# Dense stage of a three-stage kernel: first product two steps ahead of the second, row scaling in two parts, counts tile by tile

## The chip, the cores and the metric

The kernel runs on one core of one Trainium2 chip. The metric is the device time of one execution in microseconds (us). A core has a matrix engine (TensorE, PE in the rows), a vector engine (VectorE, DVE), a scalar engine (ScalarE, ACT), a general one (GpSimd, POOL) and queues for transfers; each runs its own list of instructions in order, and they wait for each other by semaphores. A bank is one of eight accumulator areas that TensorE writes.

## The reference

Three parts follow each other: a gated linear recurrence over 768 positions for 4 x 8 heads, a mixture of eight experts (top one), and a dense layer. The change touches only the last:

```python
def _moe2_ref(x, w_in, w_out) -> np.ndarray:      # x (3072, 320), w_in (320, 2048), w_out (2048, 320)
    h = x @ w_in
    g = np.maximum(0.01 * h, h)
    return (g @ w_out).astype(np.float32)
```

Its input is the experts' output, and its result is the output of the whole, 3072 rows of 320 float32 numbers.

## The kernel before

**Numbers in two halves.** Products are made with float16 operands. A float32 operand is split in a high half (its float16 rounding) and a low half (the rest), and three of the four partial products are summed in a bank: high by high, high by the weights' low half, low by high. Rows of x are first divided by a power of two of their size, so that halves keep their bits, and the result is multiplied by its inverse (`yinv`) at the end.

**Tiles and steps.** The 3072 rows are 24 tiles of 128 rows, in 6 groups (`NGR`) of 4 tiles (`GT`). The 2048 hidden columns are 16 steps (`2 * NF`) of 128. In a step f of a group:

- TensorE, `f_first`: first product, 8 matmuls over 512 columns (the group's rows), into `bank[f % 2]`; the rows say L1514.
- ACT, `group`: 0.01 times the bank into `ft` (L856).
- DVE, `group`: maximum of bank and `ft` into `fgl` (L1315).
- ACT: high half `fhi` from `fgl` (L860).
- DVE: low half `flo`, `fgl` minus `fhi` (L1320).
- TensorE, `f_second`: second product, for each of the 4 tiles 3 matmuls over 320 columns, summed over all steps in `bank[4]` to `bank[7]` (L1649).

`ft`, `fgl`, `fhi` and `flo` have two buffers each, by f % 2. In the traces' names `ft`, `fgl`, `yh`, `yl` and `ob` lie in "stage", `fhi` in "dec", `flo` and the scaled rows `ysc` in "qk".

**Order.** It is written by hand on each engine. TensorE issues first product f and then second product f - 1. At the border of two groups the last second product of the old group comes behind first product 0 of the new. After the last second product of a group ACT copies the four banks out with `rows_out` (L873, four instructions, one wait ahead of them), and the second product of step 0 waits for all four. POOL then scatters each tile's rows to the output by an indirect transfer (L627).

**Preparing the next group.** While group gr runs, the four tiles of group gr + 1 are made ready at the steps of `PREP_AT`: DVE's `y_scale` (L1295 to L1300: the rows' largest magnitude, five on one number per row, and two that scale the rows) stands between the maximum and the low half of step f; in the next step TensorE transposes the tile (`y_turn`, L1625, 3 matmuls) behind the second product, ACT takes the high half (`y_high`, L847) and DVE the low half (`y_low`, L1305). The last group has no such work.

**Counts.** `f_h`, `f_t`, `f_g`, `f_hi`, `f_lo` and `f_o` count first products, leaky parts, maxima, high halves, low halves and second products; `f_ob` counts output rows, by tiles.

Of the kernel before, what the change touches and what calls it, by code (L numbers as in the profile page):

```python
# [26 lines left out]
I32 = mybir.dt.int32  # L27
U32 = mybir.dt.uint32
ALU = mybir.AluOpType
ACT = mybir.ActivationFunctionType  # L30
AX = mybir.AxisListType
ds = bass.ds
# [14 lines left out]
NPAIR = NST + NE - 1  # L47
KR = DM - 2 * P
NF = FE // P
NU = NE + 2  # L50
GT = 4
NGR = NST // GT
# [3 lines left out]
POW_X = 2.0  # L56
# [8 lines left out]
def build(nc, qkT, k_in, v_in, o_in, ig, fg, wg_in, wA, wB, out):  # L65
    ctx = ExitStack()
    with ctx:
# [128 lines left out]
        m_h, m_hh, m_hl, m_o, m_y = sem("m_h"), sem("m_hh"), sem("m_hl"), sem("m_o"), sem("m_y")  # L196

        ys_chain, ys_done, f_tr, f_yh, f_yl = sem("ys_chain"), sem("ys_done"), sem("f_tr"), sem("f_yh"), sem("f_yl")
# [52 lines left out]
        Y = xreg[:, :].rearrange("p (t d) -> p t d", t=NST)  # L251
# [6 lines left out]
        sxt = sb("sxt", [P, 8], F32)  # L258
# [22 lines left out]
        def part(s, k):  # L281
# [1 line left out]
            if k < 3:  # L283
                return stA[s][:, k * FE:(k + 1) * FE]
            return stB[s][:, (k - 3) * NF // 2 * DM:(k - 2) * NF // 2 * DM]

        def pow2(dve, link, src, sc, inv, top):

            link(nc.vector.tensor_scalar(sc, src, 1e-30, 1e30, ALU.max, ALU.min))
            link(nc.vector.tensor_scalar(sc.bitcast(I32), sc.bitcast(I32), 0x7F800000, None, ALU.bitwise_and))  # L290
            nc.vector.tensor_scalar(inv, sc, 1.0 / top, None, ALU.mult)
            link(nc.vector.reciprocal(sc, sc))
            return nc.vector.tensor_scalar(sc, sc, top, None, ALU.mult)


        def row_of(eng, x):

# [337 lines left out]
        def _(act):  # L635
            a = nc.scalar
# [213 lines left out]
            def group(gr, i, prep):  # L850
                for f in range(2 * NF):
                    n = gr * 2 * NF + f
                    act.wait_ge(f_h, n + 1)
                    if not (isinstance(n, int) and n < 2):
                        act.wait_ge(f_g, n - 1)
                    a.activation(ft[f % 2], bank[f % 2][:, :], ACT.Copy, scale=0.01).then_inc(f_t, 1)  # L856
                    act.wait_ge(f_g, n + 1)
                    if not (isinstance(n, int) and n < 2):
                        act.wait_ge(f_o, n - 1)
                    a.copy(fhi[f % 2], fgl[f % 2]).then_inc(f_hi, 1)  # L860
                    if f == 0 and not (isinstance(gr, int) and gr == 0):
                        rows_out(gr - 1, 1 - i)
                    if prep and f - 1 in PREP_AT:
                        q = PREP_AT.index(f - 1)
                        y_high((gr + 1) * GT + q, 1 - i, q)

            def rows_out(gr, i):

                act.wait_ge(f_o, (gr + 1) * 2 * NF)
                if gr >= 2:  # L870
                    act.wait_ge(ob_free[i], 16 * GT // 2 * (gr - i))
                for q in range(GT):
                    a.activation(ob[i][:, q * DM:(q + 1) * DM], bank[4 + q][:, 0:DM], ACT.Copy,  # L873
                                 scale=yinv[:, ds(gr * GT + q, 1)]).then_inc(f_ob, 1)

# [8 lines left out]
        def _(dve):  # L884
# [397 lines left out]


            def y_scale(t, q):
                if not (isinstance(t, int) and t < 2):
                    dve.wait_ge(f_tr, t - 1)
                k = [0]

                def lk(ins):
                    k[0] += 1  # L1290
                    ins.then_inc(ys_chain, 1)
                    dve.wait_ge(ys_chain, t * YS_LINKS + k[0])

                yt = Y[:, ds(t, 1), :].rearrange("p a d -> p (a d)")
                lk(v.tensor_reduce(sxt[:, 0:1], yt, AX.X, ALU.max, apply_absolute_value=True))  # L1295
                lk(pow2(dve, lk, sxt[:, 0:1], sxt[:, 1:2], sxt[:, 2:3], POW_X))
                v.tensor_scalar(ysc[q % 2][:, 0:DM], yt, sxt[:, 1:2], None, ALU.mult)
                v.tensor_scalar(ysc[q % 2][:, DM:3 * P], Y[:, ds(t, 1), 2 * P:DM].rearrange("p a d -> p (a d)"),
                                sxt[:, 1:2], None, ALU.mult)
                v.tensor_tensor(yinv[:, ds(t, 1)], sxt[:, 2:3], winvp[:, NE:NE + 1], ALU.mult).then_inc(ys_done, 1)  # L1300
                assert k[0] == YS_LINKS, k[0]
# [7 lines left out]
            def group(gr, i, prep):  # L1309
                for f in range(2 * NF):  # L1310
                    w = gr * 2 * NF + f
                    dve.wait_ge(f_t, w + 1)
                    if not (isinstance(w, int) and w < 2):
                        dve.wait_ge(f_lo, w - 1)
                    v.tensor_tensor(fgl[f % 2], bank[f % 2][:, :], ft[f % 2], ALU.max).then_inc(f_g, 1)  # L1315
                    if prep and f in PREP_AT:
                        q = PREP_AT.index(f)
                        y_scale((gr + 1) * GT + q, q)
                    dve.wait_ge(f_hi, w + 1)
                    v.tensor_tensor(flo[f % 2], fgl[f % 2], fhi[f % 2], ALU.subtract).then_inc(f_lo, 1)  # L1320
                    if prep and f - 1 in PREP_AT:
                        q = PREP_AT.index(f - 1)
                        y_low((gr + 1) * GT + q, 1 - i, q)


# [23 lines left out]
        def _(pe):  # L1349
# [288 lines left out]
            def f_second(gr, f):  # L1638
                w = gr * 2 * NF + f
                pe.wait_ge(f_lo, w + 1)  # L1640
                if f == 0:
                    if isinstance(gr, int) and gr == 0:
                        pe.wait_ge(m_y, NPAIR + 1)
                    else:
                        pe.wait_ge(f_ob, gr * GT)
                for q in range(GT):
                    for z, (x, hl_) in enumerate(((fhi, 0), (fhi, 1), (flo, 0))):
                        c0 = (2 * (f % NF) + hl_) * DM
                        ins = t_.matmul(bank[4 + q][:, 0:DM], x[f % 2][:, q * P:(q + 1) * P],  # L1649
                                        slotB[2 + f // NF][:, c0:c0 + DM], start=(f == 0 and z == 0),  # L1650
                                        stop=(f == 2 * NF - 1 and z == 2))
                ins.then_inc(f_o, 1)

            def group(gr, i, prep):
                for f in range(2 * NF):
                    f_first(gr, f, i)
                    if f == 0 and not (isinstance(gr, int) and gr == 0):
                        f_second(gr - 1, 2 * NF - 1)
                    if f:
                        f_second(gr, f - 1)  # L1660
                    if prep and f - 1 in PREP_AT:
                        q = PREP_AT.index(f - 1)
                        y_turn((gr + 1) * GT + q, q)


# [12 lines left out]
                group(gr, 1, True)  # L1678
                group(gr + 1, 0, True)
            group(NGR - 1, 1, False)  # L1680
            f_second(NGR - 1, 2 * NF - 1)

# [12 lines left out]
NSL = 5  # L1697
XS_LINKS = 4
YS_LINKS = 5
PREP_AT = [2, 5, 8, 11]  # L1700
IN_PER_STEP = 16 * 8
HALF_ROW, BIG_ROW = -(P / 2 - 0.25), P * 1.5 * 2.0 ** 23

# [124 lines left out]
```

## Time and profile before

| | us |
|---|---|
| Median of three runs (lowest, highest) | 857.47 (855.05, 863.86) |
| The profiled execution, its own time | 860.35 |
| Its span in the trace | 858.6 |
| TensorE busy, page | 754.0 |
| First product of the dense stage starts | 497.15 |
| Last second product of the stage starts | 844.61 |

The page shows one execution. Busy time of matmuls is modelled: each is given a latency, so neighbours overlap in the rows, and the distance of two starts is what one costs. A row of the timeline has start and length in us, engine, line, operation, output and inputs, and in brackets how long the engine was idle before it and what ended that idleness. Rows of a list of waits have the total wait, how often, and the longest. The granted clock is given as a share of full speed.

### The profile page before, as it was taken

The page shows a single profiled execution, that of the slowest core. Times are in us where ns is not written, and L with a number is a line of the kernel's source. Part 1 is how long each engine was busy: PE and PEld are TensorE (multiplying, and loading weights), DVE is VectorE, ACT ScalarE, POOL GpSimd, SP SyncE. Part 2 cuts the span into 40 slices and gives each one's busy share as a digit, 9 for nine tenths or more (in the row PEclk, how much of TensorE's full clock was granted, in tenths as well). Part 3 has the DMA queues.
Part 4 walks back from the last instruction along what each step waited for, and adds up shares of the span by engine and source line. Part 5 has one row for each costly group of instructions (what it writes and reads, how often), then busy time and mean ns, then how long its engine had stood idle before and what let it go on. Part 6 is the DMA issues. An engine that isn't in the chain of part 4 may idle for free.

```text
span 858.6 us, 17692 instructions
## 1 busy us (share of the span) xinstructions
PE 754.0 (88%) x6435; PEld 553.7 (64%) x6436; DVE 535.2 (62%) x1406; ACT 391.2 (46%) x713; POOL 146.7 (17%) x202
## 2 busy tenths in 40 slices
PE   0789999998278899999999899999999999999993
PEld 0577887886167788888888755555555555555552
DVE  6468998896957556765567745455455454454341
ACT  2457474572526366554546233343433433434331
POOL 4334343443031111111100000010100100100101
PEclk9999999999589899999999999999999999999998
DMA  9569999991063983679420000000000000000000
GB/s 237 136 163 304 286 302 304 272 236 60 0 197 140 358 294 111 232 256 349 136 73 2 2 1 1 1 32 1 23 9 1 31 0 0 31 0 1 32 1 31
DMA packets 49401, 99.75 MB, mean 116 GB/s; under 512 B 7822, under 2 KB 38222, under 8 KB 46766
## 3 DMA queue, kind: packets, MB, share of 16 engines
q1 hardware_dynamic: 39906, 67.65, 26.4%
q10 hardware_dynamic: 6780, 22.10, 7.5%
q0 software_dynamic: 2640, 9.01, 3.1%
q8 instruction: 46, 0.75, 0.4%
q14 instruction: 29, 0.24, 0.1%
HBM read 74.85 MB, written 23.89 MB: 115 GB/s over the span
## 4 chain that ended last, share of the span: by engine, by line
PE 69%; DVE 12%; issue 7%; DMA 4%; ACT 4%; SPq 1%; POOL 1%; DVEq 0%; ACTq 0%
PE bank L1514 26%; PE bank L1649 13%; PE bank L1548 11%; PE bank L1381 4%; PE bank L1410 4%; ACT stage L856 2%; DVE qk L1320 2%; DMA vv<-v_in 2%; PE bank L1402 1%; PE bank L1394 1%; PE bank L1433 1%; DMA d_parts<-xreg 1%; DVE stage L1315 1%; DVE sxt L1295 1%; PE bank L1504 1%
## 5 line engine op out<-in xcount | busy, mean ns | idle before, releaser
L1514 PE MATMUL bank<-stage,slot 128*128 128x512 f16 x768 | 181.3, 379 | 0.0
L1649 PE MATMUL bank<-slot,dec 128*128 128x320 f16 x768 | 159.3, 299 | 15.7 <-DVE qk L1320 13.0
L1514 PE MATMUL bank<-qbd,slot 128*128 128x128 f16 x1984 | 122.3, 225 | 11.9 <-issue 11.7
L1315 DVE TENSOR_TENSOR stage<-bank,stage 128x512 f32<-128x512 f32 x96 | 66.4, 692 | 105.2 <-ACT stage L856 98.3
L1514 PEld LDWEIGHTS bank<-qbd,slot 128*128 128x128 f16 x1984 | 118.2, 101 | 15.4 <-issue 15.0
L1514 PEld LDWEIGHTS bank<-stage,slot 128*128 128x128 f16 x768 | 75.2, 98 | 74.1
L856 ACT ACTIVATE stage<-bank 128x512 f32<-128x512 f32 x96 | 57.5, 599 | 128.6 <-PE bank L1514 126.9
L1649 PEld LDWEIGHTS bank<-slot,dec 128*128 128x128 f16 x768 | 73.0, 98 | 66.9 <-DVE qk L1320 23.7
L1649 PE MATMUL bank<-slot,qk 128*128 128x320 f16 x384 | 114.8, 299 | 0.0
L1548 PE MATMUL bank<-slot,emov 128*128 128x320 f16 x496 | 102.0, 299 | 2.3 <-issue 1.5
L1320 DVE TENSOR_TENSOR qk<-stage,dec 128x512 f16<-128x512 f32 x96 | 66.3, 691 | 52.1 <-ACT dec L860 52.1
L860 ACT CAST dec<-stage 128x512 f16<-128x512 f32 x96 | 59.5, 620 | 73.3 <-DVE stage L1315 72.6
L627 POOL DMA_INDIRECT out<-stage,tok_i x24 | 23.6, 985 | 392.5 <-ACT stage L873 388.5
L803 ACT ACTIVATE emov<-bank 128x512 f16<-128x512 f32 x62 | 36.8, 597 | 92.0 <-PE bank L1514 85.9
L1548 PE MATMUL bank<-slot,esta 128*128 128x320 f16 x248 | 74.2, 299 | 0.0
L981 DVE SCALAR_TENSOR_TENSOR slot<-stage,wsc,slot 128x1024 f16<-128x1024 f32 (+2 forms) x50 | 69.2, 1393 | 0.4
L1235 DVE SCALAR_TENSOR_TENSOR esta<-bank,emov 128x512 f16<-128x512 f32 x62 | 42.3, 690 | 43.3 <-ACT emov L803 42.8
L742 ACT ACTIVATE dec<-bank 128x384 f32<-128x384 f32 (+1 forms) x72 | 32.6, 454 | 72.6 <-PE bank L1373 72.3
L709 ACT ACTIVATE slot<-stage,wsc 128x1024 f16<-128x1024 f32 (+1 forms) x50 | 59.7, 1227 | 2.3 <-DVE winvp L962 2.3
L1548 PEld LDWEIGHTS bank<-slot,emov 128*128 128x128 f16 x496 | 47.0, 98 | 19.7 <-issue 3.1
L988 DVE TENSOR_TENSOR dec<-bank,dec 128x384 f32<-128x384 f32 (+1 forms) x72 | 36.3, 505 | 20.0 <-PE bank L1381 16.3
L1649 PEld LDWEIGHTS bank<-slot,qk 128*128 128x128 f16 x384 | 37.6, 98 | 14.6
(261 smaller groups left out, 1133.5 us busy)
## 6 DMA issues: line engine op xcount, KB each, us to landing
slot<-d_w SPq DMA_DIRECT2D x12, 1280.0 KB, 6.7
d_w<-slot ACTq DMA_DIRECT2D x4, 2560.0 KB, 9.8
stage<-wB SPq DMA_DIRECT2D x6, 1280.0 KB
stage<-wA SPq DMA_DIRECT2D x6, 1024.0 KB
d_w<-slot SPq DMA_DIRECT2D x4, 1280.0 KB, 8.3
stage<-wB ACTq DMA_DIRECT2D x4, 1280.0 KB
qk<-qkT SPq DMA_DIRECT2D x12, 360.0 KB
slot<-qkT SPq DMA_DIRECT2D x12, 360.0 KB
```

The costliest lines, as they stand in the source:

```text
L709: a.activation(o_, t, ACT.Copy, scale=sc).then_inc(hi_done, 1)
L803: a.activation(hh[i][:, q * 512:(q + 1) * 512], bank[2 * i + q][:, :], ACT.Relu).then_inc(m_hh, 1)
L856: a.activation(ft[f % 2], bank[f % 2][:, :], ACT.Copy, scale=0.01).then_inc(f_t, 1)
L860: a.copy(fhi[f % 2], fgl[f % 2]).then_inc(f_hi, 1)
L981: v.scalar_tensor_tensor(o_, x, sc, h_, ALU.mult, ALU.subtract).then_inc(lo_done, 1)
L988: v.tensor_tensor(dec[i][:, 0:w], psS[i][:, 0:w], dec[i][:, 0:w], ALU.mult).then_inc(p_done, 1)
L1235: v.scalar_tensor_tensor(hl[i][:, q * 512:(q + 1) * 512], bank[2 * i + q][:, :], 0.0, hh[i][:, q * 512:(q + 1) * 512], ALU.max, ALU.subtra ...
L1315: v.tensor_tensor(fgl[f % 2], bank[f % 2][:, :], ft[f % 2], ALU.max).then_inc(f_g, 1)
L1320: v.tensor_tensor(flo[f % 2], fgl[f % 2], fhi[f % 2], ALU.subtract).then_inc(f_lo, 1)
L1514: ins = t_.matmul(pf, a[:, col:col + P], x(k), start=(q == 0), stop=(q == len(ops) - 1))
L1548: ins = t_.matmul(bank[4 + i][:, 0:DM], x[i][:, f * P:(f + 1) * P], slotB[s][:, c0:c0 + DM], start=(f == 0 and q == 0), stop=(f == NF - 1 ...
L1649: ins = t_.matmul(bank[4 + q][:, 0:DM], x[f % 2][:, q * P:(q + 1) * P], slotB[2 + f // NF][:, c0:c0 + DM], start=(f == 0 and z == 0), stop ...
```

## The change

- TensorE: second product f - 2 follows first product f (f - 1 before). At a border, the last two second products of the old group follow first products 0 and 1 of the new; behind the last group two second products are left.
- ACT: `rows_out` of the old group moves from behind the high half of step 0 to between the leaky part and the high half of step 1, and waits for each tile of the last second product by itself. The high half of step f waits, as before, for second product f - 2 (now counted in tiles).
- TensorE: each tile's last matmul of a second product counts `f_o` (before: the last of all four), and second product 0 waits for `f_ob` tile by tile.
- DVE: `y_scale` is cut in `y_top` (the largest magnitude, between maximum and low half) and `y_unit` (the rest, behind the low half). The helper `pow2` goes; of its five instructions the last multiplication goes, and the reciprocal is taken of the divided number.
- `PREP_AT` moves from steps 2, 5, 8, 11 to 1, 4, 7, 10, and transposes, high and low halves follow two steps later (`TURN`), in the same steps 3, 6, 9, 12 as before.

```diff
--- before.py
+++ after.py
@@ scalar engine @@
                     a.activation(ft[f % 2], bank[f % 2][:, :], ACT.Copy, scale=0.01).then_inc(f_t, 1)
+                    if f == 1 and not (isinstance(gr, int) and gr == 0):
+                        rows_out(gr - 1, 1 - i)
                     act.wait_ge(f_g, n + 1)
                     if not (isinstance(n, int) and n < 2):
-                        act.wait_ge(f_o, n - 1)
+                        act.wait_ge(f_o, GT * (n - 1))
                     a.copy(fhi[f % 2], fgl[f % 2]).then_inc(f_hi, 1)
-                    if f == 0 and not (isinstance(gr, int) and gr == 0):
-                        rows_out(gr - 1, 1 - i)
-                    if prep and f - 1 in PREP_AT:
+                    if prep and f - TURN in PREP_AT:
...
             def rows_out(gr, i):
-                act.wait_ge(f_o, (gr + 1) * 2 * NF)
                 if gr >= 2:
                     act.wait_ge(ob_free[i], 16 * GT // 2 * (gr - i))
                 for q in range(GT):
+                    act.wait_ge(f_o, GT * ((gr + 1) * 2 * NF - 1) + q + 1)
@@ vector engine @@
+            def y_top(t):
+                lk = y_link(t, [0])
+                lk(v.tensor_reduce(sxt[:, 0:1], Y[:, ds(t, 1), :].rearrange("p a d -> p (a d)"), AX.X, ALU.max,
+                                   apply_absolute_value=True))
+            def y_unit(t, q):
+                if not (isinstance(t, int) and t < 2):
+                    dve.wait_ge(f_tr, t - 1)
+                k = [1]
+                lk = y_link(t, k)
+                lk(v.tensor_scalar(sxt[:, 0:1], sxt[:, 0:1], 1e-30, 1e30, ALU.max, ALU.min))
+                lk(v.tensor_scalar(sxt[:, 0:1].bitcast(I32), sxt[:, 0:1].bitcast(I32), 0x7F800000, None, ALU.bitwise_and))
+                lk(v.tensor_scalar(sxt[:, 2:3], sxt[:, 0:1], 1.0 / POW_X, None, ALU.mult))
+                lk(v.reciprocal(sxt[:, 1:2], sxt[:, 2:3]))
                 yt = Y[:, ds(t, 1), :].rearrange("p a d -> p (a d)")
-                lk(v.tensor_reduce(sxt[:, 0:1], yt, AX.X, ALU.max, apply_absolute_value=True))
-                lk(pow2(dve, lk, sxt[:, 0:1], sxt[:, 1:2], sxt[:, 2:3], POW_X))
                 v.tensor_scalar(ysc[q % 2][:, 0:DM], yt, sxt[:, 1:2], None, ALU.mult)
...
                     v.tensor_tensor(fgl[f % 2], bank[f % 2][:, :], ft[f % 2], ALU.max).then_inc(f_g, 1)
                     if prep and f in PREP_AT:
-                        q = PREP_AT.index(f)
-                        y_scale((gr + 1) * GT + q, q)
+                        y_top((gr + 1) * GT + PREP_AT.index(f))
                     dve.wait_ge(f_hi, w + 1)
                     v.tensor_tensor(flo[f % 2], fgl[f % 2], fhi[f % 2], ALU.subtract).then_inc(f_lo, 1)
-                    if prep and f - 1 in PREP_AT:
-                        q = PREP_AT.index(f - 1)
+                    if prep and f in PREP_AT:
+                        q = PREP_AT.index(f)
+                        y_unit((gr + 1) * GT + q, q)
+                    if prep and f - TURN in PREP_AT:
+                        q = PREP_AT.index(f - TURN)
                         y_low((gr + 1) * GT + q, 1 - i, q)
@@ tensor engine @@
                 for q in range(GT):
+                    if f == 0 and not (isinstance(gr, int) and gr == 0):
+                        pe.wait_ge(f_ob, (gr - 1) * GT + q + 1)
                     for z, (x, hl_) in enumerate(((fhi, 0), (fhi, 1), (flo, 0))):
...
-                ins.then_inc(f_o, 1)
+                    ins.then_inc(f_o, 1)
             def group(gr, i, prep):
                 for f in range(2 * NF):
                     f_first(gr, f, i)
-                    if f == 0 and not (isinstance(gr, int) and gr == 0):
-                        f_second(gr - 1, 2 * NF - 1)
-                    if f:
-                        f_second(gr, f - 1)
-                    if prep and f - 1 in PREP_AT:
+                    if f < 2 and not (isinstance(gr, int) and gr == 0):
+                        f_second(gr - 1, 2 * NF - 2 + f)
+                    if f >= 2:
+                        f_second(gr, f - 2)
+                    if prep and f - TURN in PREP_AT:
...
-            f_second(NGR - 1, 2 * NF - 1)
+            for f in range(2 * NF - 2, 2 * NF):
+                f_second(NGR - 1, f)
...
-PREP_AT = [2, 5, 8, 11]
+PREP_AT = [1, 4, 7, 10]
+TURN = 2
```

TensorE in the middle of a group, before. A first product into bank0 (an even step) is followed by a second product that reads buffer 1 (dec1 is the high half, qk1 the low one), so that of the step before:

```order
L1514 MATMUL bank0<-stage,slot3 128x512 [waits f_g]
L1514 MATMUL bank0<-stage,slot3 128x512 x7
L1649 MATMUL bank4<-slot3,dec1 128x320 [waits f_lo]
L1649 MATMUL bank4<-slot3,dec1 128x320
L1649 MATMUL bank4<-slot3,qk1 128x320
```

The same place in the changed kernel:

```order
L1524 MATMUL bank0<-stage,slot3 128x512 [waits f_g]
L1524 MATMUL bank0<-stage,slot3 128x512 x7
L1658 MATMUL bank4<-slot3,dec0 128x320 [waits f_lo]
L1658 MATMUL bank4<-slot3,dec0 128x320
L1658 MATMUL bank4<-slot3,qk0 128x320
```

The second product now reads the buffer of the same parity, that of two steps before.

DVE in a step with row scaling, before (first row: maximum; last but one: low half; last: the next step's maximum):

```order
L1315 TENSOR_TENSOR stage<-bank,stage 128x512
L1295 TENSOR_REDUCE sxt<-xreg 128x1
L289 TENSOR_SCALAR sxt<-sxt 128x1
L290 TENSOR_SCALAR sxt<-sxt 128x1
L291 TENSOR_SCALAR sxt<-sxt 128x1
L292 RECIPROCAL sxt<-sxt 128x1
L293 TENSOR_SCALAR sxt<-sxt 128x1
L1297 TENSOR_SCALAR qk<-xreg,sxt 128x320
L1298 TENSOR_SCALAR qk<-xreg,sxt 128x64
L1300 TENSOR_TENSOR yinv<-sxt,winvp 128x1
L1320 TENSOR_TENSOR qk<-stage,dec 128x512
L1315 TENSOR_TENSOR stage<-bank,stage 128x512
```

And in the changed kernel:

```order
L1323 TENSOR_TENSOR stage<-bank,stage 128x512
L1291 TENSOR_REDUCE sxt<-xreg 128x1
L1327 TENSOR_TENSOR qk<-stage,dec 128x512
L1300 TENSOR_SCALAR sxt<-sxt 128x1
L1301 TENSOR_SCALAR sxt<-sxt 128x1
L1302 TENSOR_SCALAR sxt<-sxt 128x1
L1303 RECIPROCAL sxt<-sxt 128x1
L1305 TENSOR_SCALAR qk<-xreg,sxt 128x320
L1306 TENSOR_SCALAR qk<-xreg,sxt 128x64
L1308 TENSOR_TENSOR yinv<-sxt,winvp 128x1
L1323 TENSOR_TENSOR stage<-bank,stage 128x512
```

Of the nine instructions between maximum and low half one stays there, seven stand behind the low half, and one is gone.

ACT where a group begins, before (high half of step 0, the old group's rows, leaky part and high half of step 1):

```order
L860 CAST dec<-stage 128x512 [waits f_o,f_g]
L873 ACTIVATE stage<-bank,yinv 128x320 [waits ob_free1,f_o]
L873 ACTIVATE stage<-bank,yinv 128x320 x3
L856 ACTIVATE stage<-bank 128x512 [waits f_g,f_h]
L860 CAST dec<-stage 128x512 [waits f_o,f_g]
```

And in the changed kernel (high half of step 0, leaky part of step 1, rows, high half of step 1):

```order
L853 CAST dec<-stage 128x512 [waits f_o,f_g]
L847 ACTIVATE stage<-bank 128x512 [waits f_g,f_h]
L864 ACTIVATE stage<-bank,yinv 128x320 [waits f_o,ob_free1]
L864 ACTIVATE stage<-bank,yinv 128x320 [waits f_o] x3
L853 CAST dec<-stage 128x512 [waits f_o,f_g]
```

The rows moved behind the leaky part of step 1, ahead of its high half, and each has its own wait.

## Rows read from the trace of the kernel before

**Rows 1.** The page, span and busy time of the engines.

```profile
span 858.6 us, 17692 instructions
PE 754.0 (88%) x6435; PEld 553.7 (64%) x6436; DVE 535.2 (62%) x1406; ACT 391.2 (46%) x713; POOL 146.7 (17%) x202
```

**Rows 2.** Waits from 500 us on: total us, times, longest.

```profile
PE bank L1649 <- DVE qk L1320: 13.0, 22, 1.2
...
PE bank L1649 <- ACT stage L873: 2.6, 5, 0.6
```

**Rows 3.** Timeline, TensorE in two steps, the second with row scaling.

```profile
641.35 0.43 PE L1649 MATMUL bank<-slot,dec 128*128 128x320 f16 x2
...
642.98 1.89 PE L1514 MATMUL bank<-stage,slot 128*128 128x512 f16 x8
...
644.70 0.43 PE L1649 MATMUL bank<-slot,dec 128*128 128x320 f16 x2
...
645.92 0.43 PE L1649 MATMUL bank<-slot,dec 128*128 128x320 f16 x2
...
646.33 1.89 PE L1514 MATMUL bank<-stage,slot 128*128 128x512 f16 x8
...
648.75 0.45 PE L1649 MATMUL bank<-slot,dec 128*128 128x320 f16 x2 [0.53 <-DVE qk L1320]
...
650.39 0.49 PE L1625 MATMUL bank<-ident,qk 128*128 128x128 f32 x3
...
650.72 1.89 PE L1514 MATMUL bank<-stage,slot 128*128 128x512 f16 x8
```

**Rows 4.** Timeline, ACT and DVE in the same two steps.

```profile
641.55 0.60 ACT L856 ACTIVATE stage<-bank 128x512 f32<-128x512 f32 x1 [1.25 <-PE bank L1514]
...
642.18 0.69 DVE L1315 TENSOR_TENSOR stage<-bank,stage 128x512 f32<-128x512 f32 x1 [1.29 <-ACT stage L856]
...
642.90 0.62 ACT L860 CAST dec<-stage 128x512 f16<-128x512 f32 x1 [0.76 <-DVE stage L1315]
...
643.55 0.69 DVE L1320 TENSOR_TENSOR qk<-stage,dec 128x512 f16<-128x512 f32 x1 [0.69 <-ACT dec L860]
...
646.14 0.47 DVE L1295 TENSOR_REDUCE sxt<-xreg 128x1 f32 x1
...
648.01 0.69 DVE L1320 TENSOR_TENSOR qk<-stage,dec 128x512 f16<-128x512 f32 x1
```

**Rows 5.** Timeline, start of the dense stage and end of the kernel.

```profile
497.15 3.62 PE L1514 MATMUL bank<-stage,slot 128*128 128x512 f16 x16
...
501.90 0.45 PE L1649 MATMUL bank<-slot,dec 128*128 128x320 f16 x2 [1.14 <-DVE qk L1320]
...
841.66 0.43 PE L1649 MATMUL bank<-slot,dec 128*128 128x320 f16 x2
...
844.61 0.45 PE L1649 MATMUL bank<-slot,dec 128*128 128x320 f16 x2 [1.16 <-DVE qk L1320]
...
846.46 1.79 ACT L873 ACTIVATE stage<-bank,yinv 128x320 f32<-128x320 f32 x4 [2.62 <-PE bank L1649]
847.26 0.97 POOL L627 DMA_INDIRECT out<-stage,tok_i  x1 [48.91 <-ACT stage L873]
...
851.08 0.97 POOL L627 DMA_INDIRECT out<-stage,tok_i  x1 [0.30 <-issue]
```

**Rows 6.** Timeline, one border of two groups.

```profile
616.68 1.89 PE L1514 MATMUL bank<-stage,slot 128*128 128x512 f16 x8
...
617.22 1.78 ACT L873 ACTIVATE stage<-bank,yinv 128x320 f32<-128x320 f32 x4
...
619.15 0.43 PE L1649 MATMUL bank<-slot,dec 128*128 128x320 f16 x2 [0.58 <-ACT stage L873]
```

**Rows 7.** Busy time by stretches: us, engines, PEclk (granted clock), DMA share, GB/s.

```profile
215.00:236.00 21.00, 4.90 (x60) 2.93 (x61) 19.16 (x57) 12.49 (x7) 1.35 (x2) 0.50 0.00 0
606.00:613.00 7.00, 7.00 (x44) 4.13 (x43) 3.06 (x5) 2.44 (x4) 0.00 (x0) 1.00 0.01 2
```

More of the change, by code:

```diff
@@ L285, in part @@
             return stB[s][:, (k - 3) * NF // 2 * DM:(k - 2) * NF // 2 * DM]
[L287 to L293, printed above, removed]
         def row_of(eng, x):
@@ L1284, in y_scale, with y_link @@
             def y_scale(t, q):
-                if not (isinstance(t, int) and t < 2):
-                    dve.wait_ge(f_tr, t - 1)
-                k = [0]
+                y_top(t)
+                y_unit(t, q)
+            def y_link(t, k):
                 def lk(ins):
@@ L1292, in lk @@
                     dve.wait_ge(ys_chain, t * YS_LINKS + k[0])
+                return lk
+            def y_top(t):
[11 more added lines that the diff above has]
+                lk(v.reciprocal(sxt[:, 1:2], sxt[:, 2:3]))
                 yt = Y[:, ds(t, 1), :].rearrange("p a d -> p (a d)")
-                lk(v.tensor_reduce(sxt[:, 0:1], yt, AX.X, ALU.max, apply_absolute_value=True))
-                lk(pow2(dve, lk, sxt[:, 0:1], sxt[:, 1:2], sxt[:, 2:3], POW_X))
                 v.tensor_scalar(ysc[q % 2][:, 0:DM], yt, sxt[:, 1:2], None, ALU.mult)
@@ L1316, in group @@
                     if prep and f in PREP_AT:
-                        q = PREP_AT.index(f)
-                        y_scale((gr + 1) * GT + q, q)
+                        y_top((gr + 1) * GT + PREP_AT.index(f))
                     dve.wait_ge(f_hi, w + 1)
                     v.tensor_tensor(flo[f % 2], fgl[f % 2], fhi[f % 2], ALU.subtract).then_inc(f_lo, 1)
-                    if prep and f - 1 in PREP_AT:
-                        q = PREP_AT.index(f - 1)
+                    if prep and f in PREP_AT:
+                        q = PREP_AT.index(f)
+                        y_unit((gr + 1) * GT + q, q)
+                    if prep and f - TURN in PREP_AT:
+                        q = PREP_AT.index(f - TURN)
                         y_low((gr + 1) * GT + q, 1 - i, q)
@@ L1640, in f_second @@
                 pe.wait_ge(f_lo, w + 1)
[L1641 to L1645, printed above, removed]
+                if f == 0 and isinstance(gr, int) and gr == 0:
+                    pe.wait_ge(m_y, NPAIR + 1)
                 for q in range(GT):
+                    if f == 0 and not (isinstance(gr, int) and gr == 0):
+                        pe.wait_ge(f_ob, (gr - 1) * GT + q + 1)
                     for z, (x, hl_) in enumerate(((fhi, 0), (fhi, 1), (flo, 0))):
@@ L1656, in group @@
                     f_first(gr, f, i)
-                    if f == 0 and not (isinstance(gr, int) and gr == 0):
-                        f_second(gr - 1, 2 * NF - 1)
-                    if f:
-                        f_second(gr, f - 1)
-                    if prep and f - 1 in PREP_AT:
-                        q = PREP_AT.index(f - 1)
+                    if f < 2 and not (isinstance(gr, int) and gr == 0):
[3 more added lines that the diff above has]
+                    if prep and f - TURN in PREP_AT:
+                        q = PREP_AT.index(f - TURN)
                         y_turn((gr + 1) * GT + q, q)
```

## Prediction

> **What bounds the kernel now.** I started with the page [rows 1]: TensorE (PE) is busy 88% of 858.6 us. Only the dense stage is edited in a way that can move much, so I read the waits of that stage next [rows 2]. TensorE idles there in two ways: 22 times for DVE's low half at L1320 (13.0 us), and 5 times for ACT's output rows at L873 (2.6 us). What a step costs without them stands in TensorE's own timeline [rows 3]. The first product of a step (8 matmuls, 512 columns) starts at 642.98, the second product (12 matmuls, 320 columns) at 644.70, the next first product at 646.33. So a step is 1.72 + 1.63 = 3.35 us, with no gap: TensorE bounds every step in which it isn't made to wait, and the gain to be had is the sum of the waits.
>
> The next step in the same rows is one with row scaling: first product at 646.33, second product not before 648.75 instead of 646.33 + 1.72 = 648.05, so 0.70 us lost. (The row prints 0.53: a matmul's modelled end overlaps the next start by 0.17, 646.33 + 1.89 against 648.05, so each printed idle stands for 0.17 more.) The transposes follow at 650.39 and take 0.33 to the next first product at 650.72; they are work, and stay.
>
> Why it waits is in the ACT and DVE rows of the same steps [rows 4]. I count from the end of a step's first product, t = 0 (641.35 and 644.70 for the two steps; that is where the following second product may start). Without scaling: ACT's leaky part starts at +0.20 (641.55), DVE's maximum at +0.83 (642.18), the high half on ACT at 642.90, +1.55, low half on DVE at 643.55, +2.20, done at +2.89. The second product wants it at +3.35: slack of 0.46. With scaling, DVE runs L1295 to L1300 from 646.14 on, and the low half starts only at 648.01, +3.31, done +4.00: late by the 0.70 that TensorE lost.
>
> **The change, part by part.**
>
> *Second product two behind the first.* It now follows two firsts and two seconds later: the low half is wanted at 1.63 + 1.72 + 1.63 + 1.72 = +6.70 instead of +3.35. What is late instead? The high half of step f overwrites the buffer that the second product of f-2 reads, and that product now stands behind first product f. It runs from 0 to +1.63. Its end is seen by ACT about 0.2 later (the 0.20 of the leaky part), so the high half moves from +1.55 to about +1.83 and the low half is done at about 1.83 + 0.65 + 0.69 = +3.2. Against +6.70 that leaves 3.5 us. The ring closes nowhere else: a first product needs the DVE maximum of f-2, done by about +1.5 of that step, and starts two seconds and one first later, at +4.98.
>
> *Row scaling in two parts.* The reduction (0.5 us) now lies between the maximum and the low half, while ACT makes the high half: free. The rest, from 646.14 + 0.47 to the 648.01 at which DVE is free again, 1.4 us, comes behind the low half, so it ends at about +4.6. It delays the next maximum (wanted at 3.35 + 0.83 = +4.2) by 0.4, and that step's low half by less, into 3.5 us of slack. One DVE instruction in five small ones goes, with the same five links of the chain: 0. The transposes want the scaled rows two steps on, at about +8.3: 3.7 us to spare. DVE has 6 x 0.69 and the 1.9 of scaling, 6.0 us, in three steps of 10.4 us, with one more subtraction for the transposed tile; it doesn't become the bound. The cover of this edit is that slack; without it each scaling would cost the 0.70 it does now.
>
> So all 20 scaling waits go (4 in each of 5 groups): **20 x 0.70 = 14.0 us.**
>
> *Start and end of the stage.* At the start [rows 5], 16 matmuls of two first products run from 497.15, so the second product could start at 497.15 + 2 x 1.73 = 500.61, but starts at 501.90: 1.29 lost. Now a third first product (maximum of step 0 done about 0.1 us before it is wanted, by the offsets above) fills it. At the end, the last second product could start at 841.66 + 1.63 = 843.29 and starts at 844.61: 1.32 lost. Now the second product of step 13 and that of 14 stand between it and its operand: the low half is done at +3.2, wanted at +3.26. **2.6 us**, with perhaps 0.1 kept.
>
> *Output rows tile by tile, one step later.* At a group's border [rows 6] the first product starts at 616.68, the four rows at 617.22 (1.78 us for all), and the second product, which overwrites the banks, at 619.15 instead of 618.40: 0.75. For the five borders [rows 2] has 2.6 printed, with 5 x 0.17 that is **3.5 us**. In the changed kernel ACT starts the rows at about +0.8 of step 1, four in 1.78 us as now, or in some 2.4 if the wait that now stands ahead of each keeps them from overlapping (an estimate, a third on top). They end at +2.6 to +3.2. The banks are overwritten from 1.63 + 1.72 = +3.35 on, tile by tile, and the first asks for the first row only: covered. Behind these waits on ACT stands the high half of step 1, which ends by +3.9 and its low half by +4.6, wanted at +6.70: covered. The four register waits on TensorE at this place are like those before each product in the loop's groups, whose steps [rows 3] are as long as work alone: 0.
>
> *The tail* [rows 5]. Rows start at 846.46 when all four tiles are done; the first scatter is issued at 847.26 and the fourth at 851.08, 1.27 apart, and the span ends 6.5 us after the fourth's 0.97. Counted tile by tile, the first tile is ready 3/4 of a second product earlier, 1.22; POOL's scatters are the slowest link and shift whole: **1.2 us**.
>
> *Counting.* 288 further increments on TensorE (3 for each of 96 second products). In [rows 3] the last of the four tiles of a second product, which carries the increment, lasts from 645.92 to 646.33, 0.41, and the mean tile 1.63 / 4 = 0.41. I take 0; the rounding of the starts allows up to 0.02 each, 5.8 us. The Trainium skill, "TensorE: Matmul & The Clock Gate", section "The cost: per-tile semaphore tail", speaks against this part: increments on completion serialize, at 26.3 ns each. By that the change would give back an estimated 288 x 26.3 ns = 7.6 us.
>
> **Sum:** 14.0 + 2.6 + 3.5 + 1.2 = 21.3. As a cross-check of the first three: [rows 2] has 13.0 + 2.6 = 15.6 us printed in 27 waits; with 27 x 0.17 it is 20.2, against 20.1. The profiled execution took 860.35 (span 858.6), which gives 839.0 (837.3). The median shown is 857.47, which gives 836.2. I forecast **837**.
>
> **The rivals.**
>
> *Half kept.* Something that the stage couldn't show keeps part of the waits, for instance the rows at the border once each has its own wait, or the last steps. If the borders and ends keep all they have, 6.1 us, the time is 837 + 6 = 843. For it: slacks of only 0.1 at start and end. Against: the slack of over 3 us at the 20 scalings. Chance 0.07.
>
> *The increments cost.* At the upper bound of the rows, 5.8 us: 843. The page's figure gives 844.6. For it: the output of each tile now signals. Against: equal tile lengths, and no gap behind a product that carries one now. Chance 0.06.
>
> *The change doesn't do it: the ring closes.* If the high half, now behind the second product of f-2, came so late that the low half of each step missed +6.70, the waits would only move. It takes 3.5 us more in the chain than the rows show; no single instruction of ACT or DVE there has over 0.7. Then about 857. Chance 0.04.
>
> *Slower: the clock.* TensorE would run some 329 us without a gap, which it never does in the kernel before. In this stage the granted clock is 1.00, the upper level of 2.4 GHz, also in a stretch of 7.00 busy us of 7.00 [rows 7]; it was 0.50, the lower level of 1.2 GHz, in a stretch where TensorE did little (4.90 of 21.00). So it fell with idleness and not with load, and fewer gaps speak for it. If sustained load nonetheless cut it, a mean grant of 0.94 would eat the gain (329 / 0.94 = 350), and below 0.91 (329 / 0.91 = 361.5, 32 us more) the kernel would be over 1% slower, at 868. Chance 0.03.
>
> **How the numbers follow.** The main case has 0.80. Its own range is the sum against the fastest and slowest of the runs shown: 855.05 - 21.3 = 834 and 863.86 - 21.3 = 842.5. Half kept and costly increments lie at 843 to 844.6, inside a range that goes to 846 with the same scatter. Downwards the gain is limited by the waits; 831 leaves some 2 us for a quicker part elsewhere. That leaves out less than 1 in 10 by the cases, and about 1 in 10 for a shift of the unedited part, whose runs spread by 1%. A measurement can tell this kernel from no change at about 1%, so at 848.9. The main case and the two at 843 hold 0.93; I take 0.02 off for scatter: faster 0.91, same 0.06, slower 0.03.
>
> **What would show it.** In the changed profile: steps of 3.35 us throughout the stage, 3.68 with transposes instead of 4.39; no wait of TensorE for DVE's low half and none for the rows; second product's idle near 0 instead of 15.6; stage from first to last product about 328.7 us (96 x 3.355 + 20 x 0.33) instead of 349.1; high halves starting at about +1.83; scatters starting right after the last second product's first tile, and 6.5 us from the last to the end. I'm wrong if a step without scaling grows beyond 3.36 (increments, or clock if the grant is below 1.00), if a wait for L873's successor stands at the borders, or if waits for the low half stay.

## The result and the profile after

The changed kernel took 834.56 us (median of 4 runs, 833.97 to 838.51) against 857.25 us for the kernel before (the three runs shown ahead of the prediction and one more): a ratio of 0.9746, 95% interval 0.9714 to 0.9778, or 2.5% faster. The forecast was 837 (831 to 846). A second series of the same kernel gave 835.48 us (830.00 to 840.47) and a ratio of 0.9752 (0.9703 to 0.9800).

The page of the changed kernel: span, busy time, TensorE's busy share and granted clock in 40 slices, and two groups (the first products, and the matmuls of the second product that read the high half). They answer to [rows 1] and to the idle time of [rows 2].

```profile
span 832.7 us, 17702 instructions
PE 746.0 (90%) x6435; PEld 552.7 (66%) x6436; DVE 531.0 (64%) x1382; ACT 388.3 (47%) x713; POOL 146.5 (18%) x202
...
PE   0798999898178899999999989999999999999994
...
PEclk9999999999589999999999999999999999999998
...
L1524 PE MATMUL bank<-stage,slot 128*128 128x512 f16 x768 | 181.1, 379 | 0.0
L1658 PE MATMUL bank<-slot,dec 128*128 128x320 f16 x768 | 159.1, 299 | 0.0
```

The idle time ahead of the second product was 15.7 us on the page of before and is 0.0; no wait of TensorE is left in the dense stage's list of waits. The timeline of two steps, the first with row scaling (its reduction is at 571.73), answers to [rows 3] and [rows 4]:

```profile
568.56 1.89 PE L1524 MATMUL bank<-stage,slot 128*128 128x512 f16 x8
...
570.29 0.43 PE L1658 MATMUL bank<-slot,dec 128*128 128x320 f16 x2
570.49 0.60 ACT L847 ACTIVATE stage<-bank 128x512 f32<-128x512 f32 x1 [1.00 <-PE bank L1524]
...
571.12 0.69 DVE L1323 TENSOR_TENSOR stage<-bank,stage 128x512 f32<-128x512 f32 x1 [0.82 <-ACT stage L847]
...
571.73 0.48 DVE L1291 TENSOR_REDUCE sxt<-xreg 128x1 f32 x1
571.92 1.89 PE L1524 MATMUL bank<-stage,slot 128*128 128x512 f16 x8
572.17 0.62 ACT L853 CAST dec<-stage 128x512 f16<-128x512 f32 x1 [1.09 <-PE bank L1658]
572.89 0.69 DVE L1327 TENSOR_TENSOR qk<-stage,dec 128x512 f16<-128x512 f32 x1 [0.69 <-ACT dec L853]
573.50 0.15 DVE L1300 TENSOR_SCALAR sxt<-sxt 128x1 f32<-128x1 f32 x1
...
574.79 0.68 DVE L1323 TENSOR_TENSOR stage<-bank,stage 128x512 f32<-128x512 f32 x1
...
575.27 1.89 PE L1524 MATMUL bank<-stage,slot 128*128 128x512 f16 x8
```

First products start at 568.56, 571.92 and 575.27, 3.36 and 3.35 apart, although row scaling lies between. From the end of the first product (570.29) the high half starts at +1.88, and what it waits for is now the second product (the name in brackets), as the ring in the argument wants. The low half starts at +2.60 and is done by +3.3.

The end of the kernel answers to [rows 5]:

```profile
819.84 0.45 PE L1658 MATMUL bank<-slot,dec 128*128 128x320 f16 x2
...
820.52 1.78 ACT L864 ACTIVATE stage<-bank,yinv 128x320 f32<-128x320 f32 x4 [1.46 <-PE bank L1658]
...
821.32 0.97 POOL L618 DMA_INDIRECT out<-stage,tok_i  x1 [45.46 <-ACT stage L864]
...
825.15 0.97 POOL L618 DMA_INDIRECT out<-stage,tok_i  x1 [0.30 <-issue]
```

The rows start 0.68 us after the last second product does, where they started 1.85 after it (844.61 and 846.46).

It helps to cut each profile in three: up to the first matmul of the dense stage; the stage, to the end of the last second product (its start plus 1.63); the tail. The last column but one is the median of all executions. The ratio is to executions of the kernel before in the same series, whose medians were 857.25 (changed), 857.80 (e1 to e4), 856.77 (e6 to e9), 854.87 (e5) and 857.15 us (e10, e11); so a ratio isn't the quotient of two rows of this table. Each profile is of one execution.

| kernel | before stage | stage | tail | median, us | ratio (95%) |
|---|---|---|---|---|---|
| before | 497.2 | 349.1 | 12.4 | 857.25 | |
| changed | 492.7 | 328.8 | 11.2 | 834.56 | 0.9746 (0.9714 to 0.9778) |
| e1 split only | 493.0 | 334.9 | 12.4 | 842.15 | 0.9856 (0.9827 to 0.9886) |
| e2 counts only | 491.5 | 345.6 | 11.2 | 853.58 | 0.9949 (0.9919 to 0.9980) |
| e3 split and counts | 492.1 | 331.4 | 11.2 | 837.01 | 0.9804 (0.9770 to 0.9839) |
| e4 two ahead only | 498.8 | 330.7 | 12.3 | 840.22 | 0.9818 (0.9790 to 0.9846) |
| e7 changed, one count | 495.6 | 330.7 | 12.3 | 841.28 | 0.9811 (0.9750 to 0.9871) |
| e8 changed, 768 increments | 497.3 | 328.8 | 11.2 | 833.56 | 0.9692 (0.9636 to 0.9748) |
| e9 changed, scaling whole | 488.6 | 328.8 | 11.2 | 831.31 | 0.9689 (0.9634 to 0.9745) |
| e10 changed again | 490.9 | 328.8 | 11.2 | 835.48 | 0.9752 (0.9703 to 0.9800) |
| e11 as e9, again | 494.1 | 328.8 | 11.2 | 834.77 | 0.9729 (0.9691 to 0.9766) |
| e5 before, longer chain | 490.6 | 365.6 | 12.4 | 871.31 | 1.0211 (1.0167 to 1.0255) |
| e6 changed, longer chain | 494.2 | 329.6 | 11.2 | 838.27 | 0.9765 (0.9703 to 0.9828) |

Stage and tail agree to a few hundredths where they should; the part ahead of the stage, which the experiments leave alone but for four early scalings, moves by 10 us. So the experiments are read from stage and tail. The changed stage gives 20.3 us and the tail 1.2, together 21.4 before rounding; the two profiles also differ by 4.5 us ahead of the stage, which is not the change's.

### The profile page after: what moved, and what is told of

Read it like the earlier page. It is cut to its first block, busy times and chain, and to the rows that moved or that the text cites. A ratio compares the mean times of both kernels' runs of the same rounds, so it can differ in the third digit from the quotient of the medians.

```text
span 832.7 us, 17702 instructions
## 1 busy us (share of the span) xinstructions
PE 746.0 (90%) x6435; PEld 552.7 (66%) x6436; DVE 531.0 (64%) x1382; ACT 388.3 (47%) x713; POOL 146.5 (18%) x202
## 4 chain that ended last, share of the span: by engine, by line
PE 81%; DMA 6%; DVE 5%; issue 3%; SPq 2%; ACT 1%; POOL 1%; ACTq 0%; DVEq 0%
PE bank L1524 33%; PE bank L1658 19%; PE bank L1558 12%; PE bank L1391 4%; PE bank L1420 3%; DMA vv<-v_in 2%; DMA d_parts<-xreg 1%; PE bank L1412 1%; PE bank L1514 1%; PE bank L1404 1%; PE bank L1443 1%; PE bank L1381 1%; PE bank L1383 1%; DMA d_x<-og 1%; PE bank L1635 1%
## 5 line engine op out<-in xcount | busy, mean ns | idle before, releaser
L1524 PE MATMUL bank<-qbd,slot 128*128 128x128 f16 x1984 | 120.1, 223 | 11.1 <-issue 11.1
L1524 PEld LDWEIGHTS bank<-qbd,slot 128*128 128x128 f16 x1984 | 116.2, 100 | 14.2 <-issue 13.9
L1658 PEld LDWEIGHTS bank<-slot,dec 128*128 128x128 f16 x768 | 75.1, 98 | 44.3 <-DVE qk L1327 0.2
```

The lines of the kernel that those rows point to most:

```text
L1524: ins = t_.matmul(pf, a[:, col:col + P], x(k), start=(q == 0), stop=(q == len(ops) - 1))
```

## The experiments

**One part alone, without the second step of distance.** The split of the scaling (e1), in the kernel before; `y_scale` is divided as in the change (with the one small instruction fewer), and nothing else:

```diff
                     if prep and f in PREP_AT:
-                        q = PREP_AT.index(f)
-                        y_scale((gr + 1) * GT + q, q)
+                        y_top((gr + 1) * GT + PREP_AT.index(f))
                     dve.wait_ge(f_hi, w + 1)
                     v.tensor_tensor(flo[f % 2], fgl[f % 2], fhi[f % 2], ALU.subtract).then_inc(f_lo, 1)
+                    if prep and f in PREP_AT:
+                        q = PREP_AT.index(f)
+                        y_unit((gr + 1) * GT + q, q)
```

> The kernel before with only the row scaling cut in two (largest magnitude between maximum and low half, the rest behind the low half); the second product stays one step behind the first, scaling stays at steps 2, 5, 8, 11, all counts as before. Theory A (what counts is when the low half is done): the low half of a scaling step starts at about +2.2 us after its first product's end, as in other steps, before the +3.35 at which it is wanted, so all 20 waits of 0.70 us go: 857.2 - 14.0 = 843 us. The next maximum is delayed to about +4.3 against +4.2, within the slack of 0.46. Rival B (only the second step of distance takes the waits away, since the moved part of the scaling is paid one step later): most of the 14 us stays, about 852 to 857 us.

Measured: 842.15 us, stage shorter by 14.2 us. The scaling waits are gone without any distance. Its timeline in a scaling step:

```profile
511.51 0.43 PE L1668 MATMUL bank<-slot,dec 128*128 128x320 f16 x2
...
512.95 0.47 DVE L1300 TENSOR_REDUCE sxt<-xreg 128x1 f32<-128x320 f32 x1
513.06 0.62 ACT L860 CAST dec<-stage 128x512 f16<-128x512 f32 x1 [0.76 <-DVE stage L1332]
...
513.78 0.69 DVE L1336 TENSOR_TENSOR qk<-stage,dec 128x512 f16<-128x512 f32 x1 [0.36 <-ACT dec L860]
...
515.69 0.69 DVE L1332 TENSOR_TENSOR stage<-bank,stage 128x512 f32<-128x512 f32 x1
```

The low half starts at +2.27 (511.51 to 513.78), 0.07 later than in a plain step (+2.20), since the reduction is covered by ACT's high half. The rest of the scaling doesn't delay the next maximum: it starts at +4.18, where it would have started without it (3.35 + 0.83). Rival B falls. The small instruction that goes with the split can't be the cause: in e9, below, it is gone too and the scaling is whole, and there the low half starts at +3.25, against +3.31 before, so without the second step of distance it would still come some 0.6 us late.

The counts (e2): in the kernel before, `f_o` is counted by tiles, and the second product of step 0 waits for each output row by itself (ACT's wait ahead of the high half is counted in tiles too, not shown).

```diff
-                act.wait_ge(f_o, (gr + 1) * 2 * NF)
                 for q in range(GT):
+                    act.wait_ge(f_o, GT * ((gr + 1) * 2 * NF - 1) + q + 1)
...
-                        pe.wait_ge(f_ob, gr * GT)
                 for q in range(GT):
+                        pe.wait_ge(f_ob, (gr - 1) * GT + q + 1)
...
-                ins.then_inc(f_o, 1)
+                    ins.then_inc(f_o, 1)
```

> The kernel before with only the counting tile by tile (second products' tiles, and the second product 0 waits for each output row by itself); ACT still makes the four rows behind the high half of step 0. Theory A: the five border waits (3.5 us) go, since the first tile's row is made at about 0.5 us after ACT starts, 0.6 us before the bank is overwritten, and the tail loses 1.2 us: 857.2 - 4.7 = 852.5 us. Rival B (each of the 288 more increments on TensorE costs something, up to 0.02 us each): up to 5.8 us back, 852.5 to 858 us, with second products longer than 1.63 us. Rival C (rows with a wait each take so long that the border waits stay): 856 us. By the Trainium skill, TensorE: Matmul & The Clock Gate, The cost: per-tile semaphore tail, an increment is an estimated 26.3 ns, 7.6 us in all.

Measured: stage shorter by 3.5 and tail by 1.2, median 853.58; the 22 waits for the low half stay (13.0 us in its trace, as in [rows 2]) and those for the rows are gone. Theory A; with the increments at nothing, since 3.5 is all that the borders had, and its plain steps are 3.35 to 3.36 us as before.

Both together (e3, the two edits above):

> The two single changes together (scaling in two parts, counting tile by tile), the second product still one step behind the first. Theory A: they add: 857.2 - 14.0 - 4.7 = 838.5 us; the only waits of TensorE left in the stage are 1.3 us each at its start and end. Rival B (the distance of two steps is what the gain rests on): 848 us or more.

Measured: 837.01 us; stage 331.4, shorter by 17.7, as 14.2 + 3.5. They add. Two waits are left, at 496.88 and 821.92, the start and the end:

```profile
496.88 0.45 PE L1667 MATMUL bank<-slot,dec 128*128 128x320 f16 x2 [1.13 <-DVE qk L1336]
...
821.92 0.45 PE L1667 MATMUL bank<-slot,dec 128*128 128x320 f16 x2 [1.16 <-DVE qk L1336]
```

So with these two edits in place the distance of two steps is worth 331.4 - 328.8 = 2.6 us: only the start and the end.

**The distance alone** (e4): the changed kernel with the scaling whole again and the counts as before.

```diff
                     if prep and f in PREP_AT:
-                        y_top((gr + 1) * GT + PREP_AT.index(f))
+                        y_scale((gr + 1) * GT + PREP_AT.index(f), PREP_AT.index(f))
...
-                    if prep and f in PREP_AT:
-                        y_unit((gr + 1) * GT + q, q)
...
+                act.wait_ge(f_o, (gr + 1) * 2 * NF)      # once, ahead of the four rows
...
+                        pe.wait_ge(f_ob, gr * GT)        # once, ahead of second product 0
```

The waits for single tiles go, and `f_o` is counted once for each second product (not shown).

> The changed kernel with only its two steps of distance: scaling whole again between maximum and low half (at steps 1, 4, 7, 10), second products counted once each, one wait for all output rows (still made in step 1). Theory A: the slack of 3.5 us swallows the whole scaling: 14.0 us gained; start and end 2.6 us; at the borders all rows are made from +1.8 to +3.6 and wanted at +3.35, so 0.3 us is lost five times, 2.0 of 3.5 us gained; the tail gains nothing: 857.2 - 18.6 = 838.6 us. Rival B (the split carries the gain): over 850 us, with waits of TensorE for the low half.

Measured: 840.22 us; stage 330.7, shorter by 18.4 us, tail as before (12.3). The distance alone also takes all scaling waits away; what is left is 1.8 us at five borders, 0.3 more than theory A had.

**One part taken back.** One count and one wait for the rows in the changed kernel (e7; the last two hunks of e4):

> The changed kernel with second products counted once each, as before, and one wait for all four output rows (scaling in two parts and the two steps of distance stay). Theory A (increments are free): rows made from +1.8 to +3.6 and wanted at +3.35 cost 0.3 us at each of 5 borders, 1.5 us, and the tail is 1.2 us longer: 834.6 + 2.7 = 837.3 us. Rival B (288 increments cost up to 0.02 us each): they come back, 831.5 to 837.3 us, with second products shorter than 1.63 us.

Measured: stage 330.7 and tail 12.3, so 3.0 us longer than the changed kernel (1.8 and 1.2), near theory A's 2.7; the median is 6.7 longer, of which 3.0 lie ahead of the stage in the profile, where this edit changes nothing. Why the four executions (839.94 to 844.58) were all that slow is open. The borders' waits are for ACT's rows:

```profile
611.58 0.43 PE L1659 MATMUL bank<-slot,dec 128*128 128x320 f16 x2 [0.24 <-ACT stage L864]
```

With the 0.17 of overlap that is 0.4 each. With 288 increments fewer, no step is shorter than 3.35.

Scaling whole again in the changed kernel, counts as changed (e9; the first two hunks of e4):

> The changed kernel with the row scaling whole again between maximum and low half (at steps 1, 4, 7, 10); distance and counts stay. Theory A: the low half of a scaling step is done about 1.0 us later than now and still 2.5 us before it is wanted: 834.6 us, no wait of TensorE. Rival B (the split matters with two steps of distance too): up to 14 us more, 848 us.

Measured: 831.31 us, stage 328.8, no wait. One scaling step of it, second product and low half:

```profile
521.60 0.43 PE L1655 MATMUL bank<-slot,dec 128*128 128x320 f16 x2
...
524.85 0.68 DVE L1327 TENSOR_TENSOR qk<-stage,dec 128x512 f16<-128x512 f32 x1
```

The low half starts at +3.25 and is done at +3.93, 0.6 us later than in the changed kernel and 2.8 before the +6.70. With two steps of distance the split is worth nothing. The median was 3 us below the changed kernel's, though, so both ran once more on one chip:

> The changed kernel unchanged, on one chip with the next run. Theory A (the 3 us between this kernel at 834.6 and the version with whole scaling at 831.3 lie in the part ahead of the dense stage, which no edit touches, and belong to the execution): stage 328.8 us again, the two kernels within 0.3% of each other, both between 831 and 838 us. Rival B (the difference belongs to the kernels): this one 3 us slower than the other again.

> The changed kernel with the row scaling whole between maximum and low half, once more, on the same chip as the run before this. Theory A: stage 328.8 us, time within 0.3% of the changed kernel's. Rival B (the difference of 3 us belongs to the kernels): 831 us against 834 to 835.

Measured: 835.48 and 834.77 us, stage 328.8 in both. The 3 us did not come back; theory A. In the profiles of e9 and e11, which are one kernel, the part ahead of the stage took 488.6 and 494.1 us.

**More increments** (e8): a further semaphore, for which nobody waits, is counted by the other two matmuls of each tile's three.

```diff
+                        if z < 2:
+                            ins.then_inc(spare, 1)
                     ins.then_inc(f_o, 1)
```

> The changed kernel with a further increment (of a semaphore that nobody waits for) on each of the other matmuls of every second product that starts a tile's sum of three: 8 more for each of 96 products, 768 in all. Theory A (increments ride along): 834.6 us, second products 1.63 us as before. Rival B (each costs up to 0.02 us by the rounding of the rows): up to 15 us more, 850 us. By the Trainium skill, TensorE: Matmul & The Clock Gate, The cost: per-tile semaphore tail, 768 x 26.3 ns is an estimated 20 us more.

(The edit has 8 increments more in each second product, two for each tile; the words of the expectation say this less clearly.) Measured: 833.56 us, stage 328.8. Tiles start 0.41 apart, with three increments each as with one:

```profile
602.46 0.43 PE L1659 MATMUL bank<-slot,dec 128*128 128x320 f16 x2
...
602.87 0.43 PE L1659 MATMUL bank<-slot,dec 128*128 128x320 f16 x2
...
603.27 0.43 PE L1659 MATMUL bank<-slot,dec 128*128 128x320 f16 x2
...
603.68 0.43 PE L1659 MATMUL bank<-slot,dec 128*128 128x320 f16 x2
...
604.09 1.89 PE L1525 MATMUL bank<-stage,slot 128*128 128x512 f16 x8
```

768 increments cost less than 0.05 us together. Rival B falls.

**The slack itself.** One more DVE instruction of 0.6 us (into unused memory; the result is untouched) ahead of each low half, in both kernels (e6 changed, e5 before):

```diff
                     dve.wait_ge(f_hi, w + 1)
+                    v.tensor_tensor(xw[:, 0:512], fgl[f % 2], fgl[f % 2], ALU.max)
                     v.tensor_tensor(flo[f % 2], fgl[f % 2], fhi[f % 2], ALU.subtract).then_inc(f_lo, 1)
```

> The changed kernel with one more DVE instruction (a maximum of 128 x 512 numbers into unused memory, about 0.6 us) between the high half's end and the low half, in each of 96 steps. Theory A (slack of 3.5 us): only the last second product waits, about 0.6 us: 835.2 us. Rival B (the chain or DVE itself is near its limit): 0.2 us or more a step, 854 us and up.

Measured: stage 329.6, 0.8 longer; the one wait is the last second product's, at 822.19 for 0.46 + 0.17, and the first second product starts 0.16 late. The other 94 swallow the instruction. (The median, 838.27, is 3.7 above the changed kernel's; 1.6 of it lie ahead of the stage in its profile and 0.8 in the stage, and the rest is within the scatter of the executions, 835.13 to 840.10.)

> The kernel before with the same further DVE instruction of about 0.6 us ahead of each low half. Theory A (slack of 0.46 us in a step without scaling, none in the others): 76 steps lose about 0.2 us each and 20 steps 0.6 us each, about 27 us more: 884 us. Rival B (the low half isn't what the second product waits for in unscaled steps, or is far from it): only the 20 steps, the start and the end lose, 13 us more: 870 us.

Measured: 871.31 us, stage 365.6: 16.5 us longer, not 27. Theory A had the mechanism and the wrong sum, rival B is 13. First products in its timeline:

```profile
639.95 1.89 PE L1515 MATMUL bank<-stage,slot 128*128 128x512 f16 x8
...
643.30 1.89 PE L1515 MATMUL bank<-stage,slot 128*128 128x512 f16 x8
...
646.87 1.89 PE L1515 MATMUL bank<-stage,slot 128*128 128x512 f16 x8
...
651.65 1.89 PE L1515 MATMUL bank<-stage,slot 128*128 128x512 f16 x8
```

The distances are 3.35, 3.57 and 4.78 (3.36, 3.36 and 4.39 before). Of the plain steps only every other is longer, by 0.21. A second product that starts 0.21 late also moves the next one's due time by 0.21, since it stands ahead of it; the next low half then has 0.46 + 0.21 of slack, which covers the added instruction. So here a wait costs once in two steps, not in each. I had charged 76 plain steps 0.2 us each, where 31 show it. The same holds in the scaling steps: where the step before had waited, they are 0.39 longer (4.78 against 4.39), and where it had not, 0.60 (4.99).

## Why the prediction was right

*Scaling waits, 20 x 0.70 = 14.0.* e1 measured 14.2 for them alone (one of the 20 was 0.86 long). The two parts of the edit that take them away do so each alone: the split in e1, the distance in e4 and e9. Here the prediction had a wrong step, which didn't move its number: it put the gain to the distance, and said of the split that without the slack of the distance each scaling would cost the 0.70 it does now. In e1 it cost 0. The prediction's own offsets gave that, a low half at +2.2 against +3.35.

*Start and end, 2.6.* 331.4 - 328.8 = 2.6 (e3 against the changed kernel). The margin of 0.1 that I feared for was just enough: the low half of the last step is done at 819.78, and its second product starts at 819.84, 0.44 after the tile before it instead of 0.41.

*Borders, 3.5.* e2: 3.5. ACT's four rows with a wait each took 1.78 us, as without, so they kept overlapping; the 2.4 allowed for was not needed.

*Tail, 1.2.* 12.36 - 11.19 = 1.2.

*Increments, 0 with a bound of 5.8.* e8 puts 768 of them below 0.05 us. The Trainium skill's 26.3 ns for each ("TensorE: Matmul & The Clock Gate", "The cost: per-tile semaphore tail"), an estimated 7.6 us here, is not borne out for increments within a stream of matmuls; no run here shows the tail behind a last matmul that the section is about.

*Offsets.* High half at +1.83, measured +1.88; low half done at +3.2, measured +3.3; rest of the scaling done at +4.6, next maximum measured at 574.79, +4.50.

*Sum.* 21.3 against 20.27 + 1.16 = 21.4 in the profile. The stage took 328.8 us, 328.7 forecast. The medians differ by 22.7, the interval of the ratio means 19.0 to 24.5. The forecast of 837 was 2.4 high: it stood 0.8 above the median less the sum (836.2, to allow for the profiled run's 839.0), and the remaining 1.6 is less than what the part ahead of the stage moves by from one execution to the next.

*The slower rival.* In the changed kernel's stretch from 600 to 700 us TensorE is busy for 100.00 us of 100.00 at a granted clock of 1.00, the level of 2.4 GHz:

```profile
600.00:700.00 100.00, 100.00 (x606) 59.59 (x604) 55.07 (x130) 41.37 (x75) 7.78 (x8) 1.00 0.04 14
```

## What to carry to other kernels

Where one engine bounds a stage and waits at a few known steps, first write down for a plain step when each operand is ready and when it is wanted: an extra job may fit in a gap of its own engine (the reduction under ACT's cast), and then no deeper pipeline is needed. A deeper pipeline and a better placed job can each take the same wait away, so their gains don't add: split plus counts gave 18.9 us in stage and tail, distance alone 18.5, all three 21.4. Check a buffer ring for the wait that a deeper pipeline adds (here the high half behind the second product of two steps before) and don't charge a late operand in each step: the second product that waits also moves the due time of the next one behind it, so in e5 the wait was paid in every other step.

## What the runs showed of the hardware that I had not expected

The part ahead of the dense stage took 488.6 to 498.8 us with nearly the same instructions. Part of it lies at one place of the expert loop, where TensorE waits near 280 us and has 64 matmuls behind the wait. The wait and the matmuls, and the stretch's busy times with the granted clock (third number from the end), in the kernel before:

```profile
281.65 6.44 PE L1514 MATMUL bank<-qbd,slot 128*128 128x128 f16 x64 [3.40 <-issue]
...
280.00:288.00 8.00, 6.34 (x65) 6.35 (x66) 1.71 (x3) 0.60 (x1) 0.38 (x1) 0.57 1.02 341
```

in e2:

```profile
280.06 3.74 PE L1514 MATMUL bank<-qbd,slot 128*128 128x128 f16 x64 [3.40 <-issue]
...
280.00:288.00 8.00, 7.47 (x91) 6.14 (x91) 4.32 (x10) 4.76 (x7) 0.11 (x1) 1.00 1.02 297
```

and in e9, with 64 matmuls of the same line some 11 us earlier as well:

```profile
268.27 5.37 PE L1521 MATMUL bank<-qbd,slot 128*128 128x128 f16 x64 [1.90 <-issue]
...
278.89 3.74 PE L1521 MATMUL bank<-qbd,slot 128*128 128x128 f16 x64 [1.66 <-issue]
...
280.00:288.00 8.00, 7.70 (x102) 6.59 (x100) 6.07 (x12) 4.75 (x7) 1.27 (x1) 1.00 1.02 292
```

After a wait of 3.40 us the granted clock was 0.57 in the stretch in one trace, mostly its lower level of 1.2 GHz, and the 64 matmuls took 6.44 us; after a wait of the same 3.40 us it was 1.00 in another, the level of 2.4 GHz, and they took 3.74. So the wait's length alone doesn't decide it, and what the lower level cost here is 2.7 us. The 13 traces fall in three groups:

| traces | 64 matmuls some 11 us earlier, us | the wait, us | the 64 behind it, us | part ahead of the stage, us |
|---|---|---|---|---|
| before, e4, e7, e8 | 3.7 | 3.20 to 3.40 | 6.4 to 6.5 | 495.6 to 498.8 |
| e1, e2, e3, e6, e11 | 3.7 | 3.21 to 3.43 | 3.7 | 491.5 to 494.2 |
| changed, e5, e9, e10 | 5.3 to 5.4 | 1.66 to 1.80 | 3.7 | 488.6 to 492.7 |

e9 and e11, one kernel, are in two of the groups, so it goes at least in part by the execution and not by the edit. What the wait is for the rows don't say ("issue"), no run tried it, and why the third group is the shortest, though its earlier 64 matmuls are slower, stays open too. It is where this kernel still loses time that none of these edits touch.
